# Gated linear attention and two MLPs on one core: the level of one token summed by VectorE, with tokens as rows

## The reference

```
f = sigmoid(f_logit)
for t in range(768):
    state = f[t][:, None] * state + outer(k[t], v[t])      # 48 x 48, for each of 32 heads
    y[t] = q[t] @ state
h = x @ w_in                     # 384 -> 2048
g = where(h >= 1, h, where(h <= -1, 0, (h + 1)**2 / 4))
x = g @ w_out                    # 2048 -> 384
out = (silu(x @ w_gate) * (x @ w_val)) @ w2_out             # 384 -> 1536 -> 384
```

## Time and profile before

| | |
|---|---|
| median of 3 runs | 1041.09 us (1040.33 to 1041.56) |
| profiled execution, own time | 1040.47 us |
| its span, first to last instruction | 1038.7 us |
| busy PE / DVE / ACT / POOL | 998.0 / 489.3 / 477.8 / 427.0 us |
| mean granted TensorE clock | 0.984 |
| on the chain that ended last | PE 91%, DVE 4%, issue 2% |

### The profile page before, as it was taken

The page is one execution under the profiler, slowest core; times in us unless marked ns, Lnnn a source line. Parts: engine busy times, 40 slices in busy tenths (PEclk is TensorE's granted clock), DMA queues, the critical chain, the costliest instruction groups (busy, mean ns, idle before and its releaser), DMA issues.

```text
span 1038.7 us, 19593 instructions
## 1 busy us (share of the span) xinstructions
PE 998.0 (96%) x8088; PEld 829.7 (80%) x8088; DVE 489.3 (47%) x622; ACT 477.8 (46%) x880; POOL 427.0 (41%) x360
## 2 busy tenths in 40 slices
PE   4787899999999999999999999999999999999997
PEld 4666688888888888888888888888888888888886
DVE  7877856844954785485346422223222232232221
ACT  4766667667666765866355422222222222221211
POOL 7657654762764475275256211221122112211121
PEclk9888999999999999999999999999999999999999
DMA  9360015006002400400531010010100100000000
GB/s 354 121 249 35 2 43 190 25 3 223 32 2 94 162 2 17 148 32 3 183 122 50 13 61 1 1 61 1 33 29 0 62 1 1 31 1 1 31 1 30
DMA packets 17368, 63.51 MB, mean 61 GB/s; under 512 B 1920, under 2 KB 2176, under 8 KB 16512
## 3 DMA queue, kind: packets, MB, share of 16 engines
q1 hardware_dynamic: 17280, 62.27, 16.5%
HBM read 52.82 MB, written 9.44 MB: 60 GB/s over the span
## 4 chain that ended last, share of the span: by engine, by line
PE 91%; DVE 4%; issue 2%; DMA 1%; ACT 1%; SPq 0%; POOL 0%; POOLq 0%; ACTq 0%; DVEq 0%
PE acc L529 11%; PE acc L530 11%; PE acc L531 11%; PE bank L557 7%; PE bank L555 7%; PE bank L556 7%; PE hid L515 7%; PE hid L516 6%; PE hid L517 6%; PE bank L386 5%; PE hid L557 2%; PE hid L555 2%; PE hid L556 2%; DVE scores L881 2%; PE bank L442 1%
## 5 line engine op out<-in xcount | busy, mean ns | idle before, releaser
L1069 POOL TENSOR_TENSOR g_lo<-prod,g_hi 128x512 fp32r<-128x512 f32 x72 | 93.0, 1292 | 347.5 <-ACT g_hi L766 347.5
L1062 POOL TENSOR_TENSOR g_lo<-act_tmp,g_hi 128x512 fp32r<-128x512 f32 x96 | 126.8, 1321 | 171.1 <-ACT g_hi L727 171.1
L965 DVE TENSOR_TENSOR sig<-sig,bank 128x512 f32<-128x512 f32 x72 | 49.5, 688 | 275.4 <-ACT sig L760 275.4
L766 ACT CAST g_hi<-prod 128x512 fp32r<-128x512 f32 x72 | 44.7, 621 | 247.8 <-PE acc L531 247.8
L1028 POOL TENSOR_TENSOR keys<-keys,gates 128x512 f32<-128x512 f32 x82 | 108.5, 1323 | 74.7 <-PE bank L386 44.9
L515 PE MATMUL hid<-x_hi,win_hi 128*128 128x512 f32 x288 | 116.8, 406 | 3.3 <-DVE act_tmp L953 2.0
L529 PE MATMUL acc<-g_hi,wout_hi 128*128 128x512 f32 x288 | 115.8, 402 | 0.0
L530 PE MATMUL acc<-g_lo,wout_hi 128*128 128x512 f32 x288 | 113.4, 394 | 0.0
L531 PE MATMUL acc<-g_hi,wout_lo 128*128 128x512 f32 x288 | 113.2, 393 | 0.0
L517 PE MATMUL hid<-x_hi,win_lo 128*128 128x512 f32 x288 | 113.2, 393 | 0.0
L516 PE MATMUL hid<-x_lo,win_hi 128*128 128x512 f32 x288 | 113.1, 393 | 0.0
(11 more groups left out here) (88 smaller groups left out, 1968.9 us busy)
## 6 DMA issues: line engine op xcount, KB each, us to landing
gates<-in_f_dram SPq DMA_DIRECT2D x12, 512.0 KB, 5.0
queries<-in_q_dram SPq DMA_DIRECT2D x12, 512.0 KB, 4.7
keys<-in_k_dram SPq DMA_DIRECT2D x12, 512.0 KB, 4.7
values<-in_v_tok_dram SPq DMA_DIRECT2D x6, 1024.0 KB, 7.7
q_tok<-in_q_tok_dram SPq DMA_DIRECT2D x12, 384.0 KB, 8.2
k_tok<-in_k_tok_dram SPq DMA_DIRECT2D x12, 384.0 KB, 8.3
x_dram<-x_out SPq DMA_DIRECT2D x6, 768.0 KB, 3.2
x_raw<-x_dram SPq DMA_DIRECT2D x6, 768.0 KB, 5.5
```

What stands on the lines that cost most here:

```text
L1062: pool.tensor_tensor(g_lo[:, c % RING, :], act_tmp[:, 2 + c % 2, :], g_hi[:, c % RING, :].bitcast(F32), ALU.subtract).then_inc(g_lo_done, 1)
```

## The change

For units a >= 2 (`APART`), four units of six, level m = 1 leaves PE:

- not issued any more: `copy_right` of steps 0 and 1 on ACT, `level` of steps 0 and 1 on PE, and the count of bank fills and copies is adapted (`apart`, `fill`, `copied`);
- SP loads two more arrays with tokens as rows into `q_tok`, each in two groups: the next token's gate logit (`fn`) after `diag_done` of the unit and ahead of `load_q`, and the next token's query (`qn`) behind `load_v`, after `next_keyed`. `load_tok` of the next unit waits for `next_done` as well;
- ACT takes the sigmoid of the first (`next_gate`, h = -7, -6), POOL multiplies it into `k_tok` (`next_key`, h = -6, -5), DVE multiplies by the next query (`next_own`, h = 0, 1) and sums the 48 numbers of each head (`next_sum`, h = 1, 2) into a new tile `nexts`;
- DVE places these sums in `scores` with two predicated copies for a group (`place_nexts`, at the h where `take_level` was), whose data come from `nexts` in SBUF instead of a PSUM bank;
- `scale_k` of steps 0 and 1 waits for the keys' load and the gates alone, `scale_q` of steps 0 and 1 no longer for the copy.

```diff
+    p = Plan(own=(-13, -12), diag=(-11, -10), next_gate=(-7, -6), next_key=(-6, -5), next_own=(0, 1), next_sum=(1, 2),
...
+def apart(a):
+    return 2 if a >= APART else 0
+
 def fill(a, i):
-    return a * FILLS + i
+    return a * FILLS + max(i, apart(a)) - sum(apart(b) for b in range(a + 1))
...
         def load_tok(a, gs=(0, 1)):
             if a > 0:
                 sp.wait_ge(diag_done, 2 * a)
+            if a > APART:
+                sp.wait_ge(next_done, 2 * (a - APART))
...
+        def load_next_gates(a):
+            sp.wait_ge(diag_done, 2 * (a + 1))
+            for g in range(2):
+                sp.dma_start(tok_group(q_tok, g), tok_group(fn[a], g)).then_inc(fn_in[g], 16)
+
+        def load_next_queries(a):
+            sp.wait_ge(next_keyed, 2 * (a - APART + 1))
+            for g in range(2):
+                sp.dma_start(tok_group(q_tok, g), tok_group(qn[a], g)).then_inc(qn_in[g], 16)
...
         for a in range(1, UNITS):
+            if a >= APART:
+                load_next_gates(a)
             load_q(a)
...
             load_v(a)
+            if a >= APART:
+                load_next_queries(a)
             if a + 1 < UNITS:
                 load_tok(a + 1)
...
             for s in placed(PLANS[a].step, h):
-                level(a, s)
+                if s >= apart(a):
+                    level(a, s)
...
+        def next_gate(a, g):
+            act.wait_ge(fn_in[g], 16 * (a - APART + 1))
+            t = tok_group(q_tok, g)
+            act.activation(t, t, ACT.Sigmoid).then_inc(next_gates, 1)
...
+        def next_own(a, g):
+            dve.wait_ge(qn_in[g], 16 * (a - APART + 1))
+            dve.wait_ge(next_keyed, 2 * (a - APART) + g + 1)
+            t = tok_group(q_tok, g)
+            dve.tensor_tensor(t, t, tok_group(k_tok, g), ALU.mult).then_inc(next_owned, 1)
+
+        def next_sum(a, g):
+            dve.wait_ge(next_owned, 2 * (a - APART) + g + 1)
+            dve.tensor_reduce(nexts[:, g * BP:(g + 1) * BP], tok_group(q_tok, g).rearrange("p (x d) -> p x d", d=D),
+                              AXIS_X, ALU.add).then_inc(next_done, 1)
+
+        def place_nexts(a, g):
+            dve.wait_ge(next_done, 2 * (a - APART) + g + 1)
+            dve.wait_ge(diag_placed, B * a + 2 * (g + 1))
+            for half in range(2):
+                o = group(scores, g)[rows(half), :, :, half * HALF:(half + 1) * HALF]
+                o = o.rearrange("p x e (b s r) -> p (x e) b s r", s=2, r=1)[:, :, :, 1, :]
+                i = nexts[rows(half), g * BP:(g + 1) * BP].rearrange("p (x b r) -> p x b r", b=1, r=1)
+                last = dve.copy_predicated(o, level_mask(0, half), i.broadcast_to([HALF, BP, HALF // 2, 1]))
+            last.then_inc(dve_took, 1)
...
         def scale_k(a, s):
-            if s < STEPS:
+            if s < apart(a):
+                pool.wait_ge(k_in[g], 16 * (a + 1))
+            elif s < STEPS:
                 pool.wait_ge(filled, fill(a, s + 1))
...
+        def next_key(a, g):
+            pool.wait_ge(next_gates, 2 * (a - APART) + g + 1)
+            t = tok_group(k_tok, g)
+            pool.tensor_tensor(t, t, tok_group(q_tok, g), ALU.mult).then_inc(next_keyed, 1)
```

More of the change, by code:

```diff
@@ L63 @@
 H_FIRST = -13
-Plan = namedtuple("Plan", "own diag place sigmoid gated copy step take block_take scale turn whole whole_take last last_take "
+Plan = namedtuple("Plan", "own diag next_gate next_key next_own next_sum place sigmoid gated copy step take block_take scale turn whole whole_take last last_take "
                           "decay y y_out tk tk_out kv state state_place")
-FIRST = Plan(own=(20, 22), diag=(20, 22), place=(21, 21, 23, 23), sigmoid=(-6, -5), gated=(-6, -4),
+FIRST = Plan(own=(20, 22), diag=(20, 22), next_gate=(), next_key=(), next_own=(), next_sum=(),
+             place=(21, 21, 23, 23), sigmoid=(-6, -5), gated=(-6, -4),
              copy=(-6, -4, 1, 3, 5, 7, 9, 11, 13, 15, 17, 19), step=(0, 2, 4, 6, 8, 10, 12, 14, 16, 18),
@@ L76, in usual @@
     two = [h for h in levels for _ in range(2)]
-    p = Plan(own=(-13, -12), diag=(-11, -10), place=(-9, -8, -6, -4), sigmoid=(-2, -1), gated=(-1, 0),
+    p = Plan(own=(-13, -12), diag=(-11, -10), next_gate=(-7, -6), next_key=(-6, -5), next_own=(0, 1), next_sum=(1, 2),
+             place=(-9, -8, -6, -4), sigmoid=(-2, -1), gated=(-1, 0),
              copy=[h + g - 2 for h in levels for g in range(2)] + [whole - 1] * 2, step=two,
@@ L87 @@
 SECOND = usual((6, 9, 12, 14, 16), 18, 21, 23, own=(-8, -8), diag=(1, 1), place=(2, 3, 4, 5), sigmoid=(-2, -1),
-               gated=(-1, 1))
+               gated=(-1, 1), next_gate=(), next_key=(), next_own=(), next_sum=())
 USUAL = usual((2, 5, 8, 11, 13), 16, 19, 21)
@@ L112, in turns, with copied @@
     return now
+def apart(a):
+    return 2 if a >= APART else 0
 def fill(a, i):
-    return a * FILLS + i
+    return a * FILLS + max(i, apart(a)) - sum(apart(b) for b in range(a + 1))
+def copied(a, n):
+    return a * COPIES + n - sum(apart(b) for b in range(a + 1))
 def scaled(a, n):
@@ L127, in merges, with build @@
     return sum(SCALES if 0 < b < UNITS - 1 else SCALES - 2 for b in range(a)) + s
-def build(nc, f, q, k, qt, kt, v, w_in, w_out, w_gate, w_val, w2_out, masks, ident, x1, out):
+def build(nc, f, q, k, qt, kt, fn, qn, v, w_in, w_out, w_gate, w_val, w2_out, masks, ident, x1, out):
     ctx = ExitStack()
@@ L203, in build @@
     qt_in, kt_in = ([sem(f"{n}_in{g}") for g in range(2)] for n in ("qt", "kt"))
+    fn_in, qn_in = ([sem(f"{n}_in{g}") for g in range(2)] for n in ("fn", "qn"))
     v_in = sem("v_in")
@@ L215, in build @@
     own_done, diag_done, diag_placed = sem("own_done"), sem("diag_done"), sem("diag_placed")
+    next_gates, next_keyed, next_owned, next_done = sem("next_gates"), sem("next_keyed"), sem("next_owned"), sem("next_done")
     state_decayed, state_placed = sem("state_decayed"), sem("state_placed")
@@ L693, in attention @@
                     take_last(a, e)
+            for g in placed(PLANS[a].next_gate, h):
+                next_gate(a, g)
             for s in placed(PLANS[a].copy, h):
-                copy_right(a, s)
+                if s >= apart(a):
+                    copy_right(a, s)
             for b in placed(PLANS[a].y_out, h):
@@ L852, in scale_q @@
             m = LEVELS[li]
-            if s < COPIES:
-                dve.wait_ge(q_copied, a * COPIES + s + 1)
-            else:
+            if apart(a) <= s < COPIES:
+                dve.wait_ge(q_copied, copied(a, s + 1))
+            elif s >= COPIES:
                 dve.wait_ge(filled, fill(a, Y0))
@@ L918, in attention @@
                 gated(a, g)
+            for g in placed(PLANS[a].next_own, h):
+                next_own(a, g)
+            for g in placed(PLANS[a].next_sum, h):
+                next_sum(a, g)
             for s in placed(PLANS[a].take, h):
-                take_level(a, s)
+                if s < apart(a):
+                    place_nexts(a, s)
+                else:
+                    take_level(a, s)
             for s in placed(PLANS[a].scale, h):
@@ L1040, in attention @@
                     own(a, g)
+                for g in placed(PLANS[a].next_key, h):
+                    next_key(a, g)
             for s in placed(PLANS[a].turn, h):
@@ L1154 @@
     laid = [("f", _by_dims(inputs["f_logit"])), ("q", _by_dims(inputs["q"])), ("k", _by_dims(inputs["k"])),
-            ("q_tok", _by_tokens(inputs["q"])), ("k_tok", _by_tokens(inputs["k"])), ("v_tok", _apart(inputs["v"])),
+            ("q_tok", _by_tokens(inputs["q"])), ("k_tok", _by_tokens(inputs["k"])),
+            ("f_next", _by_tokens(_next(inputs["f_logit"]))), ("q_next", _by_tokens(_next(inputs["q"]))), ("v_tok", _apart(inputs["v"])),
             ("w_in", _in_pieces(inputs["moe_w_in"])), ("w_out", _out_pieces(inputs["moe_w_out"])),
```

16 lines of the change are left out of this document (11 added, 5 removed).

## The result

The changed kernel takes 1057.7 us in the median (1057.15 to 1059.15, 4 runs) against 1040.71 us (1040.05 to 1041.56, 4 runs) of the kernel before: ratio 1.0167, 95% interval 1.0155 to 1.0179. It is slower, by 17.0 us. Its profiled execution took 1059.15 us, with a span of 1057.4 us.

The account below looks back on a forecast made before the run. PE was taken to bound the kernel; DVE's 7.3 us delay less 1.60 slack shifts each unit 5.7 us, four units 22.8, giving 1064 us. Range 1058 to 1068 us, chance 0.47; wide range 1047 to 1076; slower in all 0.83.

Parts of the forecast that it names:

- What bounds and what can be won: PE sets the time in units 2 to 5; removing the level saves 2.24 us a unit, 8.96 us at most.
- DVE's new work: Two products and two sums add 3.5 us a unit on DVE; idle gaps absorb 2.15; the four copies keep 5.43 us.
- Rival 1: The new placing copies on DVE take only 0.70 us each: +12.5 us, 1053.6 us; chance 0.14.
- The turns: DVE and POOL hold each other on SBUF: placing copies held 3.75 us a unit, `scale_q` pairs +1.2 and +1.25.
- Rival 2: The placing copies are not held by POOL, or POOL's work falls elsewhere: +7.8 us, 1048.9 us; chance 0.10.
- The sum: DVE's delay at `activate` of chunk 2: 7.5 us by terms, 7.3 taken; PE starts `hidden` of chunk 4 5.7 us later.
- the slack of 1.60: Before the change, DVE's maximum of MLP chunk 2 ends 1.60 us before `hidden` of chunk 4 needs it.
- inner forecast of 1058 to 1068: Whole kernel takes 1058 to 1068 us with DVE late by 6 to 8.5 us a unit; chance 0.47.
- The signs: Expected in the profile: PE waits of 1 to 3 us, copies 1.36 us or 2.4 to 2.9 beside POOL, period 95 us.
- the two named: Places where PE was to wait 1 to 3 us: `hidden` of chunk 3 and of chunk 4, MLP units 1 to 4.
- The rest: Added ACT sigmoids, POOL products and SP loads cost nothing; otherwise up to 1.6, 1.9 and 1.5 us a unit.
- rival 4: PE's clock falls to half behind waits, +1.4 us a unit, or late queries +1.5: 1070 us; chance 0.12.

## Why the prediction was right, point by point

**What bounds and what can be won.** Right. PE was full, the level cost 2.24 us a unit, and the removal shows as such wherever VectorE is out of the way: in the run with sums in their own buffer and PSUM the start of `hid` moves ahead by 2.24 us at each level's place.

**DVE's new work.** Right in size: products 0.948 us, sums 0.942 us, copies 1.30 us where not held (1.36 predicted). Rival 1, copies of 0.70 us, is out: the earlier trace rows's range depends on the level. The formula of the Trainium skill ("VectorE: DVE Perf Modes", section "The TRN2 errata"), which would give 0.69 us, doesn't carry over from tensor_tensor to this instruction at level one; the measurement decides.

**The turns.** Right in kind, and shown twice: data in PSUM instead of SBUF take 2.23 us off a period, data in SBUF instead of PSUM put 2.5 on. Rival 2 is out. The Trainium skill's rule ("SBUF — State Buffer", section "SBUF: two separate sides") holds in that a PSUM source takes no part. The size was off, and it is the term that was mis-sized: the copies were put down as held for 3.75 us and cost 7.67 - 5.43 = 2.24 more than before. The prediction took the rule's whole instruction as it stands and had them pay for the whole of each GpSimd instruction. The rows show less: `g_lo` starts at 275.14, the copy in front of it ends at 276.23, and `g_lo` is done 0.96 us later, not 1.29; `scale_k` and `merge` behind it are 0.3 us short of their own time in the same way. From the end of the first copy to the end of the second are 2.13 us, where the copy and `g_lo` by themselves add up to 2.59. The measurement decides.

**The sum.** In the time of before, with TensorE 7.12 us late when unit 3's level is due (`hidden` of chunk 1 starts at 269.21 us instead of 262.09), L1025 of chunk 2 is late by 288.87 - 7.12 - 276.52 = 5.2 us; the prediction had 7.3, and 1.5 of the difference are the copies. The two pairs of `scale_q` came out close: 2.99 - 2.05 = 0.9 us more where 1.2 were put down, and 2.39 - 1.28 = 1.1 for 1.25. Less the slack of 1.60 the 5.2 give 3.6 us, and the period grew by 3.86: 5.7 was predicted. Four times the difference is 7.4 us. The forecast of 1064 us is only 6 us above the measured 1057.7, since the first period grew by 1.6 us more, which no term has. The time lies inside the wide range of 1047 to 1076 us and 0.3 us below the inner forecast of 1058 to 1068; that it comes so near to the latter is luck, as VectorE's delay of 5.2 us lies outside the 6 to 8.5 that went with it, and 1040.7 + 4 x 3.86 would be 1056.1 us. The signs were met in kind and came out smaller: copies of 1.9 to 2.3 us where held, for 2.4 to 2.9, and a period of 93.45 for 95.

**What was missed but didn't decide.** TensorE waits at four places in a unit, not at the two named. By the prediction's terms `activate` of chunk 0 is late by 3.5 - 0.52 + 1.2 = 4.2 us, against 3.8 measured (273.73 - 7.12 in the time of before, where it started at 262.83). The prediction didn't carry this on to ScalarE, where `take_x1` stands behind `g_hi`. In the changed kernel this is covered by the later waits: VectorE has no idle gap from there to chunk 4, so its delay at that place does not depend on them; in the kernels that relieve VectorE later on it is what remains.

**The rest.** The clock did not fall (rival 4). The granted clock of the stretches with the longest waits:

```profile
273.40:278.00 4.60, 2.48 (x11) 1.68 (x10) 4.59 (x5) 3.49 (x7) 2.86 (x2) 1.00 0.68 264
283.40:290.00 6.60, 5.04 (x20) 3.55 (x21) 6.55 (x7) 4.32 (x7) 5.79 (x5) 1.00 0.00 1
```

The loads, the sigmoids (0.848 us each) and the key products (1.844) cost nothing in the change, as costed. The loads of `qn` landed in 3.6 us, not 8.2 as the earlier trace rows for loads with others beside them.

**Left open.** The first of the four periods grew by 5.5 us, 1.6 more than the others. 0.7 of it stand at chunk 12 of MLP unit 0, where TensorE has one idle of 0.4 us with no releaser in the profile; every variant of the changed kernel shows something there (0.1 to 1.1 us), the one built on the kernel before does not. No run was made for it, and its cause stays open. Most of the rest goes with the wait at `hidden` of chunk 2, 1.66 us there against 1.02: in that unit the gated queries run beside a `g_lo` and take 3.26 us instead of 2.35. No version was found that beats both kernels.

## What to carry to other kernels

When the bounding engine is relieved by giving work to another one, read the other's load between two results that the bounding engine waits for, chunk by chunk; its busy share over the period (63% here) and even its load over three chunks said nothing, twice over. Moving an input from PSUM to SBUF can cost more than the instruction: count who else of VectorE and GpSimd then has two SBUF inputs in the same stretch, and count the hold on both sides. And a load that shares its buffer with an earlier step of the same chain can't be moved ahead with the work; give it a buffer first.

## What the runs showed of the hardware beyond the expected

- A predicated copy of 512 elements costs 1.30 to 1.33 us at level one, whether its data come from a PSUM bank or from a broadcast column in SBUF, and 0.74 from m = 4 on; 0.70 is the least.
- GpSimd and VectorE, with all inputs of both in SBUF, change sides at each instruction's end, even when the same engine has the next one ready. A held copy and the GpSimd instruction beside it take some 0.46 us less than the sum of both alone (2.13 us against 2.59 for a copy and `g_lo`).
- A wait of TensorE costs 0.3 to 0.4 us more than its bracket: two waits of 1.02 and 1.11 us in the run without copies made the period 90.11 - 87.36 = 2.75 us longer, 0.31 more for each, and the four of the change 0.36 more for each.
- Waits of 1.0 to 1.5 us, four in 15 us, leave the granted clock at 1.00, which is the 2.4 GHz level; one of 2.27 us before the changed part, followed by 1.26 us of matmuls of 64 columns, was followed by wide matmuls at the 1.2 GHz level: the granted clock is 0.52 from 128 to 131 us.
